# Softmax steps placed between first-layer blocks, late rows reordered, a one-pass route, and TensorE's first loop experts written out

## The reference, cut to what matters

```python
# 1 attention: 8 heads of 64, causal with decay lam, in blocks, state carried over
# 2 experts: E=8, w1[e] 512x1024, w2[e] 1024x512
for s in range(S):
    fresh_e = argmax(logits[b, s])
    e = fresh_e if s == 0 or local_gate[b, s] < 0.5 else prev_e
    p = exp(logits[b, s] - max); p /= p.sum() + 1e-9
    out[b, s] = p[e] * (relu(x[b, s] @ w1[e]) @ w2[e])
# 3 gated convolution: out = (sigmoid(conv5(x)) * (x @ w_val)) @ w_out
```

## Time and profile before

| | us |
|---|---|
| median of 3 runs | 359.69 (359.45 to 360.14) |
| the profiled execution | 360.69 |
| its span, first to last instruction | 358.9 |
| TensorE busy | 344.5 (96%) |
| VectorE busy | 235.0 (65%) |
| ScalarE busy | 176.3 (49%) |
| GpSimd busy | 71.2 (20%) |

### The profile page before, as it was taken

The page is one execution under the profiler, slowest core; times in us unless marked ns, Lnnn a source line. Parts: engine busy times, 40 slices in busy tenths (PEclk is TensorE's granted clock), DMA queues, the critical chain, the costliest instruction groups (busy, mean ns, idle before and its releaser), DMA issues.

```text
span 358.9 us, 6809 instructions
## 1 busy us (share of the span) xinstructions
PE 344.5 (96%) x2566; PEld 310.3 (86%) x2566; DVE 235.0 (65%) x505; ACT 176.3 (49%) x299; POOL 71.2 (20%) x67
## 2 busy tenths in 40 slices
PE   7999999977899999999999999999999699999997
PEld 7887888867889989899899898998988598889986
DVE  6778889977682854836729367185480779899920
ACT  2333545414263845636547357284560758577422
POOL 3624899926000000000000000000400640000000
PEclk9999999989899999999999999999999899999999
DMA  7999999334748375593773936936311540101112
GB/s 201 420 412 393 405 401 374 108 111 162 250 163 302 123 273 195 176 350 103 290 250 120 339 131 252 327 118 235 117 31 44 142 141 30 60 0 60 59 51 98
DMA packets 31146, 70.11 MB, mean 195 GB/s; under 512 B 2704, under 2 KB 3216, under 8 KB 30608
## 3 DMA queue, kind: packets, MB, share of 16 engines
q1 hardware_dynamic: 26192, 59.25, 45.7%
q0 software_dynamic: 1920, 6.29, 5.5%
q10 hardware_dynamic: 3008, 4.22, 3.2%
HBM read 55.08 MB, written 14.68 MB: 194 GB/s over the span
## 4 chain that ended last, share of the span: by engine, by line
PE 80%; DVE 7%; DMA 6%; issue 2%; ACT 2%; POOL 1%; ACTq 0%; SPq 0%; DVEq 0%; POOLq 0%
PE bank L1245 76%; DMA qkv_sb<-qkv 6%; PE bank L1403 2%; PE bank L1506 1%; DVE p_den L1042 1%; DVE scores_sb L904 1%; DVE bank L951 1%; DVE member_rank L949 1%; POOL k_scaled L494 1%; ACT w_raw L761 1%; DVE hold L948 0%; DVE x_sp L978 0%; ACT w_sp L747 0%; PE bank L1450 0%; DVE x_sp L988 0%
## 5 line engine op out<-in xcount | busy, mean ns | idle before, releaser
L1245 PE MATMUL bank<-w_sp,h_sp 128*128 128x512 f32 (+1 forms) x480 | 107.0, 381 | 0.0
L1245 PEld LDWEIGHTS bank<-w_sp,h_sp 128*128 128x128 f32 x480 | 86.4, 188 | 16.7
L1245 PE MATMUL bank<-x_sp,w_sp 128*128 128x256 f32 x768 | 95.3, 286 | 3.0 <-DVE h_sp L1072 3.0
L1245 PEld LDWEIGHTS bank<-x_sp,w_sp 128*128 128x128 f32 x768 | 94.6, 195 | 3.6 <-issue 3.1
L994 DVE TENSOR_TENSOR w_sp<-w_raw,w_sp 128x1024 fp32r<-128x1024 f32 x62 | 73.2, 1221 | 12.4 <-ACT w_sp L622 12.2
L622 ACT ACTIVATE w_sp<-w_raw 128x1024 fp32r<-128x1024 f32 x68 | 68.5, 1057 | 13.9 <-PE bank L1245 13.7
L1072 DVE SCALAR_TENSOR_TENSOR h_sp<-bank,h_sp 128x512 fp32r<-128x512 f32 x32 | 22.0, 689 | 62.6 <-ACT h_sp L661 61.2
L661 ACT ACTIVATE h_sp<-bank 128x512 fp32r<-128x512 f32 x32 | 19.1, 598 | 49.8 <-PE bank L1245 49.8
L1245 PE MATMUL bank<-w_sp 128*128 128x384 f32 x192 | 36.9, 348 | 3.1 <-issue 3.0
L1245 PEld LDWEIGHTS bank<-w_sp 128*128 128x128 f32 x192 | 34.9, 195 | 4.8 <-issue 3.6
L565 POOL DMA_INDIRECT x_all<-y_slots,early_u x3 | 3.8, 1271 | 168.9 <-DMA y_slots<-y_out 168.3
(11 more groups left out here) (144 smaller groups left out, 396.2 us busy)
## 6 DMA issues: line engine op xcount, KB each, us to landing
w_raw<-w SPq DMA_DIRECT2D x32, 1024.0 KB, 5.5
qkv_sb<-qkv SPq DMA_DIRECT2D x22, 512.0 KB, 13.5
x_slots<-zeros SPq DMA_DIRECT2D x4, 1024.0 KB, 15.2
x_in<-x_slots SPq DMA_DIRECT2D x7, 512.0 KB, 6.6
y_slots<-y_out ACTq DMA_DIRECT2D x7, 512.0 KB, 5.3
out<-x_in SPq DMA_DIRECT2D x11, 256.0 KB, 2.0
w_raw<-w_val SPq DMA_DIRECT2D x1, 1024.0 KB, 5.2
w_raw<-w_out SPq DMA_DIRECT2D x1, 1024.0 KB, 6.5
```

Source lines behind the costliest of these rows:

```text
L1245: return nc.tensor.matmul(o, lhsT, rhs, start=start, stop=stop, skip_group_check=free)
```

## The change

Seven edits:
- VectorE's softmax steps (now `probabilities`) move from ahead of expert 0 to behind `h_parts(0, 1)`. Reading n_over and the branch move behind `last_hot`.
- The half split (2, 1) of w2's first half moves from GpSimd's end to VectorE, between `h_parts(0, 0)` and `h_parts(0, 1)`; unit (3, 0) stays behind the second block and (3, 1) moves behind the third. ScalarE's order stays.
- GpSimd does `low_late(8)` and `low_late(9)` inside tile 10's round, ahead of `split_lo_half(2, 0)`, and waits for the first `hot_slots` before `low_late(10)` and `low_late(11)`.
- TensorE does all of `late_rows(8)` ahead of the last `transpose_pick`.
- The route's operands `member_rank` and `route_rhs` become float32r.
- TensorE's experts 1 and 2 are written out; its loop runs over 3 to 6.
- 14 instead of 12 warm-up products (`warm`) at the start.

```diff
--- before.py
+++ after.py
@@ -34,6 +34,7 @@
 CHUNKS = TOKENS // SEQ
 HALO = TAPS - 1
 FIRST = 3
+PEELED = 3
 LAST_AT = (E - 1) * CAP
 Q = 32
 LATE = 4
@@ -68,7 +69,7 @@
         slot_hot = sb("slot_hot", [P, 2, CAP], F32R)
         over_iota = sb("over_iota", [P, OVER, E])
         over_step = sb("over_step", [P, OVER, E])
-        route_rhs = sb("route_rhs", [Q + E, E + 2])
+        route_rhs = sb("route_rhs", [Q + E, E + 2], F32R)
         iota_col = sb("iota_col", [E, 1])
         fresh_below = sb("fresh_below", [P, 1])
         lam_all = sb("lam_all", [P, H])
@@ -94,8 +95,9 @@
         prob_e = sb("prob_e", [P, TILES, E])
         prob_sum = sb("prob_sum", [P, TILES])
         hold = sb("hold", [E, 2, P])
-        member_rank = sb("member_rank", [Q + E, 2, P])
+        member_rank = sb("member_rank", [Q + E, 2, P], F32R)
         member = member_rank[0:E]
+        member_f = member.bitcast(F32)
         rank_own = member_rank[Q:Q + E]
         route_tok = sb("route_tok", [P, TILES, E + 2])
         member_tok = route_tok[:, :, 0:E]
@@ -530,13 +532,16 @@
                     scatter(0)
                 if t >= 4:
                     scatter(t - 3)
+                if t == TILES - 2:
+                    low_late(TILES - 4)
+                    low_late(TILES - 3)
                 if half >= 0:
                     split_lo_half(half // 2, half % 2)
-            for t in range(TILES - LATE, TILES):
-                low_late(t)
+            pool.wait_ge(slot_hot_ok, 1)
+            low_late(TILES - 2)
+            low_late(TILES - 1)
             for t in range(TILES - LATE, TILES):
                 scatter(t)
-            split_lo_half(2, 1)
 
             pool.wait_ge(routed_ok, 1)
             n_over = pool.snap(pool.value_load(n_over_i[0:1, 0:1], min_val=0, max_val=OVER))
@@ -872,8 +877,8 @@
 
             nc.vector.memset(fresh_below[:, :], FRESH_BELOW)
             nc.vector.memset(pick[:, :, :], 0.0)
-            nc.vector.memset(member_rank[:, :, :], 0.0)
-            nc.vector.memset(route_rhs[:, :], 0.0)
+            nc.vector.memset(member_rank[:, :, :].bitcast(F32), 0.0)
+            nc.vector.memset(route_rhs[:, :].bitcast(F32), 0.0)
             link(nc.vector.memset(no_add[:, :], 0.0))
             dve.wait_ge(lam_in, 16)
             for s in range(2):
@@ -892,7 +897,7 @@
             nc.vector.memset(fresh_below[0:1, :], ALWAYS_FRESH)
             nc.vector.tensor_copy(route_rhs[0:E, 0:E], ident[0:E, 0:E])
             nc.vector.tensor_copy(route_rhs[0:E, E:E + 1], iota_col[:, :])
-            nc.vector.memset(route_rhs[Q:Q + E, E:E + 2], 1.0)
+            nc.vector.memset(route_rhs[Q:Q + E, E:E + 2].bitcast(F32), 1.0)
             link(nc.vector.tensor_copy(k_decay[:, :, :], decay[:, :, :, P - 1:P].rearrange("p s a o -> p a (s o)")))
             nc.vector.memset(hold[:, :, :], 0.0).then_inc(decay_ok, 1)
 
@@ -947,10 +952,10 @@
                     dve.wait_ge(route_ok, t - 1)
                 link(nc.vector.tensor_copy(hold[:, q, :], ps_pick[Q:Q + E, 0:P]))
                 link(nc.vector.tensor_tensor_scan(member[:, q, :], hold[:, q, :], ps_pick[0:E, 0:P],
-                                                  member[:, q, P - 1:P] if t >= B else 0.0, ALU.mult, ALU.add))
-                link(nc.vector.tensor_tensor_scan(rank[:, q, :], ones_ps, member[:, q, :],
+                                                  member_f[:, q, P - 1:P] if t >= B else 0.0, ALU.mult, ALU.add))
+                link(nc.vector.tensor_tensor_scan(rank[:, q, :], ones_ps, member_f[:, q, :],
                                                   rank[:, 1 - q, P - 1:P] if t else 0.0, ALU.mult, ALU.add))
-                nc.vector.tensor_tensor(rank_own[:, q, :], rank[:, q, :], member[:, q, :], ALU.mult).then_inc(rank_ok, 1)
+                nc.vector.tensor_tensor(rank_own[:, q, :], rank[:, q, :], member_f[:, q, :], ALU.mult).then_inc(rank_ok, 1)
 
             def place(t):
 
@@ -1037,17 +1042,19 @@
             link(nc.vector.tensor_reduce(n_over_f[:, :], over_n[:, :], AX_X, ALU.add))
             link(nc.vector.tensor_copy(n_over_i[:, :], n_over_f[:, :]))
 
-            dve.wait_ge(exp_ok, 1)
-            link(nc.vector.tensor_reduce(prob_sum[:, :], prob_e[:, :, :], AX_X, ALU.add))
-            link(nc.vector.tensor_scalar(p_den[:, :], prob_sum[:, :], 1e-9, None, ALU.add))
-            link(nc.vector.reciprocal(p_den[:, :], p_den[:, :]))
-            link(nc.vector.tensor_tensor(p_tmp[:, :, :], prob_e[:, :, :], member_tok[:, :, :], ALU.mult))
-            link(nc.vector.tensor_reduce(p_tok[:, :], p_tmp[:, :, :], AX_X, ALU.add))
-            link(nc.vector.tensor_tensor(p_tok[:, :], p_tok[:, :], p_den[:, :], ALU.mult))
-            nc.vector.tensor_scalar(gather_u[:, :], slot_f[:, :], float(SLOTS - 1), None, ALU.min).then_inc(routed_ok, 1)
-
-            n_over = dve.snap(dve.value_load(n_over_i[0:1, 0:1], min_val=0, max_val=OVER))
-            with dve.If(n_over > 0):
+            def probabilities():
+
+                dve.wait_ge(exp_ok, 1)
+                link(nc.vector.tensor_reduce(prob_sum[:, :], prob_e[:, :, :], AX_X, ALU.add))
+                link(nc.vector.tensor_scalar(p_den[:, :], prob_sum[:, :], 1e-9, None, ALU.add))
+                link(nc.vector.reciprocal(p_den[:, :], p_den[:, :]))
+                link(nc.vector.tensor_tensor(p_tmp[:, :, :], prob_e[:, :, :], member_tok[:, :, :], ALU.mult))
+                link(nc.vector.tensor_reduce(p_tok[:, :], p_tmp[:, :, :], AX_X, ALU.add))
+                link(nc.vector.tensor_tensor(p_tok[:, :], p_tok[:, :], p_den[:, :], ALU.mult))
+                nc.vector.tensor_scalar(gather_u[:, :], slot_f[:, :], float(SLOTS - 1), None,
+                                        ALU.min).then_inc(routed_ok, 1)
+
+            def over_places():
 
                 over_link(nc.vector.tensor_tensor_scan(over_end[:, :], ones[:, 0:E], over_n[:, :], 0.0, ALU.mult, ALU.add))
                 over_link(nc.vector.tensor_tensor(over_beg[:, :], over_end[:, :], over_n[:, :], ALU.subtract))
@@ -1081,11 +1088,17 @@
                     split_lo(i, r, (hi_ok[i], 2 * n + 1 + half), lo_ok[i])
 
                 h_parts(first, e, 0)
+                if not begun:
+                    unit(e, 2, 1)
                 h_parts(first, e, 1)
+                if not begun:
+                    probabilities()
+                unit(e, 3, 0)
                 if begun:
-                    unit(e, 3, 0)
                     unit(e, 3, 1)
                 h_parts(first, e, 2)
+                if not begun:
+                    unit(e, 3, 1)
                 unit(e + 1, 0, 0)
                 h_parts(first, e, 3)
                 if more:
@@ -1115,8 +1128,11 @@
                     nc.vector.tensor_scalar(hot[:, s, :], slot_iota[:, :], last_slot[:, s:s + 1],
                                             p_tok[:, s * B:s * B + 1], ALU.is_equal, ALU.mult).then_inc(hot_ok, 1)
 
-            expert(0, True, True)
+            expert(0, False, True)
             last_hot()
+            n_over = dve.snap(dve.value_load(n_over_i[0:1, 0:1], min_val=0, max_val=OVER))
+            with dve.If(n_over > 0):
+                over_places()
             with dve.Fori(1, E - 1) as e:
                 expert(e, True, True)
             expert(E - 1, True, False)
@@ -1352,7 +1368,7 @@
                         last.then_inc(first.xt, 1)
 
             pe.wait_ge(warm_ok, 1)
-            warm(12, ps_route)
+            warm(14, ps_route)
             pe.wait_ge(ident_ok, 2)
             for t in range(TILES):
                 scores(t)
@@ -1375,9 +1391,8 @@
             transpose_pick(TILES - 2)
             route(TILES - 3)
             early_rows()
-            late_rows(TILES - 4, (0, 1))
+            late_rows(TILES - 4)
             transpose_pick(TILES - 1)
-            late_rows(TILES - 4, (2, 3))
             route(TILES - 2)
             late_rows(TILES - 3, (0, 1))
             route(TILES - 1)
@@ -1476,7 +1491,9 @@
                     pe.wait_ge(hot_ok, s + 1)
                     last = nc.tensor.transpose(ps_hot[a][:, s * P:(s + 1) * P], hot[:, s, a * P:(a + 1) * P], ident[:, :])
                 last.then_inc(hotT_ok, 1)
-            with pe.Fori(1, E - 1) as e:
+            for e in range(1, PEELED):
+                expert(e, True, False)
+            with pe.Fori(PEELED, E - 1) as e:
                 expert(e, True, False)
             expert(E - 1, False, False)
             late_yT(1, range(DT))
```

## The result

The changed kernel took 350.31 us (median of four runs, 349.39 to 351.42), beside 359.91 us for the kernel before (359.45 to 361.14) in the same comparison: 9.6 us less, a ratio of 0.9729 with an interval of 0.9688 to 0.977.

The account below looks back on a forecast made before the run. TensorE was busy 344.5 of 358.9 us, so only its waits and half-clock stretches could give time. Gains 1.2 + 1.6 + 4.55 = 7.35, taken as 7.1: 360.69 to 353.6 profiled, median 352.6 us, range 351.5 to 355.6.

Parts of the forecast that it names:

- (h): Experts 1 and 2 written out on TensorE: 0, gain excluded; dearest end a cost of 3.00 us.
- the signs that I had named for being wrong: TensorE standing at expert 1's transposes, or gaps without a releaser in experts 1 and 2.
- (a): GpSimd's low rows reordered: first slot_hot comparison no longer held up, 0.93 to 1.2 us gained on VectorE's chain.
- (c): late_rows(8) whole before pick's last transpose: cost 0 to 0.1 us; with (a) and (b) last route 1.2 us earlier.
- (b): Route in one pass: 0 to 0.2 us saved each, about 0.15 on the last route; earlier ones mostly not counted.
- (d): Last route to expert 0's up phase: 3.1 us instead of 4.71, gain 1.6 us if the clock stays up.
- (e): Softmax behind expert 0's second block: up phase from 16.44 to 11.52 plus 0.35 us, gain 4.55 us.
- (f): Weight split moved from GpSimd to VectorE: GpSimd loses 2.44 us where little waited; VectorE's 1.22 counted in (e).
- (g): VectorE's value load and branch, 1.36 us, moved behind last_hot: cost 0.
- (i): Two more warm matmuls at the start, while TensorE waits for qkv's first load: 0.
- The clock did not fall: Rival: TensorE's clock falls all the same in the remaining gaps, losing 1.7 us, 354.2 us; chance 0.24.
- x_in of expert 1: Rival: its load ends last, 2 us too late giving 354.6; chance 0.11, shared with any other new wait.

Follow-up runs that it names:

- the experiment alone: Kernel before with only TensorE's experts 1 and 2 written out: 359.23 us beside 361.47, ratio 0.9936.
- the five with the same instructions up to there: Changed kernel; it with loop kept; with longer jump; with five experts written out; with split on GpSimd: 350.31, 353.71, 353.1, 353.66, 350.24 us.
- the two-pass route: Changed kernel with route_rhs and member_rank back in float32, two instructions a route: 351.16 us, ratio 0.9743.
- five written out: Changed kernel with five of TensorE's loop experts written out instead of two: 353.66 us, ratio 0.9836.
- The two kernels with the same TensorE instructions up to 90 us: Changed kernel with float32 route, 351.16 us; kernel before with only GpSimd's and TensorE's late-row orders changed and 14 warm products, 358.49 us.

## Why the prediction was right, and where it was wrong

**The failed step is (h)**, the term for writing out TensorE's experts, put at 0 with the sentence "A gain is excluded by the edge that costs nothing". The edge does cost nothing, in after too (22.45). But writing code out does not only remove edges; it moves all the code behind it. The row of 3.00 us at 282.76 was before me, I named it as the dearest gap that no data explain, and used it only as a price that the change might add. It was a price that the change might as well take away: the bound should have had both signs, 352.6 + 3.0 and 352.6 - 3.0 and more. The term was 3.3 in the profiles instead of 0; the experiment alone gave 2.2 and its removal 3.4 (2.8 by the ratios). All the rest of the change together, with the loop kept, took 353.71 us, inside the width of 351.5 to 353.8 that I gave the sum. None of the signs that I had named for being wrong came, since they looked at experts 1 and 2 and not behind the loop. I had also set the rule of the Trainium skill against the loop's edges alone, and not against the branch of the earlier trace rows behind which the gap stood.

**The account.** For the profiled execution I forecast 353.6, and it took 349.72, 3.9 less: 3.3 from (h), and 0.6 as the first part gave 7.7 instead of the 7.1 that I took. The median was to be 1.0 lower than the profiled time, and was 0.6 higher; that takes 1.6 of the 3.9 away again, so the error is 2.3. The 0.6 of the first part is mostly luck of the execution that was profiled: of the five with the same instructions up to there its up phase starts the earliest, and their mean start, 79.25, would make the 7.7 a 7.2.

**(a) and (c), with the last route of (b), 1.2 us**: 1.5 in the two profiles, since the last route started at 75.55, not 75.85. The working behind it missed twice. VectorE came to the first comparison at 69.78, ahead of the 70.57 at which I had GpSimd's split end; and GpSimd's queue, which I took as fixed, ran earlier too, so that the split ended at 69.88. The wait between the routes was 0.84, as forecast (0.9). Undoing (a) alone costs 1.13 us between the comparison and the last route, the upper of its two ends; but in one of the five executions with this order 0.7 us of the hold-up were still there, which my two ends did not allow for.

**(b), 0.15 us**: right for the one route on the path, 0.12 us. Whether the earlier routes count, which I had ruled out, stays open: VectorE comes to the first comparison at 69.78, and at 70.50 with the two-pass route, but the five executions with the one-pass route have it anywhere from 69.78 to 71.37.

**(d), 1.6 us**: last route to up phase 3.15 us, forecast 3.1. The size was right. Its reason was half right: with the gap of 1.88 us filled on the kernel before, the mean clock rose from 0.983 to 0.990 and 1.9 us were gained, but the clock fell in the profile all the same. That the other short gaps would leave it up I had called the uncertain part, and no run shows why they did.

**(e), 4.55 us**: right. The up phase took 11.81 (forecast 11.87); softmax ended at 87.7 (88.4), TensorE asked for it at 90.3. The part alone gave 4.3 (2.1 to 5.1 by its interval), in a profile with a longer fall of the clock in front.

**(f), (g), (i), 0**: right. The split on either engine gives the same time, the value load showed in no wait, and two warm products more changed nothing on either kernel.

**The rivals.** The clock did not fall between 71 and 98 us in after's profile, nor in seven of the eight others that have its order on TensorE and VectorE; but one of after's four runs has a mean clock of 0.995, which is what the profile of the 12 warm products has with its one fall. x_in of expert 1 was issued at 85.75 (forecast 85.9) and landed 3.6 us later, at 89.4, with 1.0 us to spare (forecast 1.2). VectorE's list held nothing else ahead of h_parts. TensorE did not starve for code in the written-out experts: the step that could have made the change slower had its sign turned.

## What to carry to other kernels

Look for gaps whose releaser is "issue" behind an engine's own branch, and treat them as a matter of where code lies: taking code out of a skipped body, or adding it ahead, can be worth 3 us or cost them, and a price bounded by such a row has both signs. Where a step of VectorE stands on the path, see to it that no GpSimd subtraction overlaps it, with room to spare: a comparison took up to 1.8 us for 0.36, and 12 elements took 2.7 us for 0.17. And put short steps on which the next stage does not depend (softmax sums, value loads, branches) behind the first blocks which that stage needs, not ahead of them.

## What the runs showed of the hardware that I had not expected

**A skip's price depends on the place.** The same branch over the same 344 instructions stood 2.65 to 3.0 us at some places and 0.3 at others, and 128 products that never run turned 0.33 into 2.80.

**A hold-up ends with GpSimd's subtraction.** In 13 of the 17 profiles the first slot_hot comparison took longer than 0.36 us, from 0.45 to 1.96. In all 13 it ended 0.15 to 0.17 us behind the end of GpSimd's last subtraction in front, wherever it had begun (before: 71.95 behind 71.79; five written out: 71.33 behind 71.16). In the other four VectorE came within 0.1 us of that end, or behind it.

**The clock's fall is not told by the idle time in front of it.** In the stretch from 71 to 83 us it fell in the profiles of all eight kernels with before's order of the softmax or of the late rows, for 3.4 or 6.8 us, with idle sums of TensorE from 0.85 us up; and in one of nine with both orders changed, though the gaps there, 1.08 and 0.84 us in after, are no shorter. The two kernels with the same TensorE instructions up to 90 us fell apart in this. Nor is a fall fixed by the kernel: the ten runs of the late rows with 14 warm products have mean clocks from 0.985 to 0.995, where 0.995 is room for one fall of 3.4 us and the profile, at 0.986, has three. Filling the gap of 1.88 us makes falls rarer; neither that gap nor the warm products are the whole cause, and what decides stays open. The Trainium skill, TensorE: Matmul & The Clock Gate, Part 1: The HAM clock gate, says that the gate's own period runs on freely and does not begin with the kernel, so that the point of a change depends on where the work falls in it. That would suit these two kernels; no run here tests it.
